# Layer 2 of a three-stage fused kernel in tiles of 1024 tokens

## The reference, cut to what matters

```python
N, C, F = 6016, 256, 2048                 # tokens, width, hidden width
qn = q / (norm(q, axis=tokens) + 1e-6);  kn = k / (norm(k, axis=tokens) + 1e-6)
a  = softmax_rows(kn.T @ qn / tau)        # 256 x 256
x  = v @ a                                # 6016 x 256
h  = x @ w_in1;   g = where(h > 0, h, exp(min(h, 0)) - 1);   x = g @ w_out1     # layer 1
h  = x @ w_in2;   g = h * sigmoid(h);                        out = g @ w_out2   # layer 2
```

## Time and profile before

| | us |
|---|---|
| time, median of 3 runs | 1018.54 (1018.07 to 1018.68) |
| the profiled execution's own time | 1018.29 |
| its span, first to last instruction | 1016.2 |
| TensorE busy in it | 1010.8 (99%) |
| VectorE busy | 790.2 (78%) |
| ScalarE busy | 572.9 (56%) |
| DMA moved | 58.86 MB, mean 58 GB/s |

### The profile page before, as it was taken

The page is one execution under the profiler, slowest core; times in us unless marked ns, Lnnn a source line. Parts: engine busy times, 40 slices in busy tenths (PEclk is TensorE's granted clock), DMA queues, the critical chain, the costliest instruction groups (busy, mean ns, idle before and its releaser), DMA issues.

```text
span 1016.2 us, 15807 instructions
## 1 busy us (share of the span) xinstructions
PE 1010.8 (99%) x5718; PEld 918.4 (90%) x5718; DVE 790.2 (78%) x1291; ACT 572.9 (56%) x926; POOL 10.2 (1%) x11
## 2 busy tenths in 40 slices
PE   9999999999999999999999999999999999999998
PEld 8888888888888888888899999999999999999998
DVE  7789878778777677776777787877878878878875
ACT  6766545555445444454445566566665665665641
POOL 0300000000000000000000000000000000000000
PEclk9999999999999999999999999999999999999999
DMA  9913202112111020110121102012022022021011
GB/s 350 367 18 73 73 24 60 63 32 73 42 21 51 13 63 41 21 57 1 42 84 73 63 1 63 16 48 62 0 62 62 0 62 62 0 62 40 14 22 37
DMA packets 109921, 58.86 MB, mean 58 GB/s; under 512 B 92208, under 2 KB 98992, under 8 KB 107056
## 3 DMA queue, kind: packets, MB, share of 16 engines
q1 hardware_dynamic: 109728, 57.95, 19.6%
q10 hardware_dynamic: 144, 0.26, 0.1%
HBM read 39.72 MB, written 18.48 MB: 57 GB/s over the span
## 4 chain that ended last, share of the span: by engine, by line
PE 98%; DMA 1%; issue 0%; DVE 0%; SPq 0%; ACT 0%; POOL 0%; DVEq 0%; POOLq 0%
PE bank L992 73%; PE bank L1124 20%; PE bank L1002 2%; PE bank L1141 2%; DMA early_w_in<-w_in 1%; PE bank L1020 0%; SPq L412 0%; ACT early_w_in_parts L341 0%; PE bank L1035 0%; PE bank L1041 0%; ACT early_scores L593 0%; DVE early_scores L787 0%; DVE small L790 0%; DVE out_tile L978 0%; SPq L489 0%
## 5 line engine op out<-in xcount | busy, mean ns | idle before, releaser
L992 PE MATMUL bank<-g_parts,w_out_parts 128*128 128x512 f32 (+1 forms) x1152 | 274.8, 375 | 0.0
L992 PE MATMUL bank<-xT_parts,a_w_in 128*128 128x512 f32 (+1 forms) x1152 | 274.3, 375 | 0.0
L992 PE MATMUL bank<-xT_parts,w_in_parts 128*128 128x512 f32 (+1 forms) x1152 | 260.6, 375 | 0.0
L652 ACT ACTIVATE g_raw<-bank 128x512 f32<-128x512 f32 (+1 forms) x192 | 112.8, 588 | 234.9 <-PE bank L992 222.1
L992 PEld LDWEIGHTS bank<-xT_parts,a_w_in 128*128 128x128 f32 x1152 | 215.7, 189 | 28.5
L992 PEld LDWEIGHTS bank<-g_parts,w_out_parts 128*128 128x128 f32 x1152 | 215.6, 189 | 28.3
L992 PEld LDWEIGHTS bank<-xT_parts,w_in_parts 128*128 128x128 f32 x1152 | 208.4, 190 | 23.5
L1124 PEld LDWEIGHTS bank<-g_pair_parts,w_out_forms 128*128 128x128 f32 x1848 | 219.9, 192 | 5.9 <-issue 1.4
L1124 PE MATMUL bank<-g_pair_parts,w_out_forms 128*128 128x256 f32 x1848 | 220.6, 275 | 1.0 <-issue 1.0
L683 ACT ACTIVATE g_pair_parts<-g_forms 128x1024 fp32r<-128x1024 f32 x88 | 93.2, 1059 | 148.0 <-DVE g_forms L902 78.9
L909 DVE TENSOR_TENSOR g_pair_parts<-g_forms,g_pair_parts 128x1024 fp32r<-128x1024 f32 x88 | 107.8, 1225 | 77.6 <-ACT g_pair_parts L683 77.6
(11 more groups left out here) (82 smaller groups left out, 401.0 us busy)
## 6 DMA issues: line engine op xcount, KB each, us to landing
y_parts<-y1T_parts SPq DMA_DIRECT2D x11, 1024.0 KB, 3.8
xT_parts<-y_parts SPq DMA_DIRECT2D x11, 1024.0 KB, 5.4
early_qk<-q SPq DMA_DIRECT2D x23, 256.0 KB, 8.0
out<-out_tile SPq DMA_DIRECT2D x45, 128.0 KB, 2.6
early_qk<-k SPq DMA_DIRECT2D x22, 256.0 KB, 8.4
v_in<-v SPq DMA_DIRECT2D x40, 128.0 KB, 3.2
early_w_in<-w_in SPq DMA_DIRECT2D x4, 512.0 KB, 10.7
early_w_out<-w_out SPq DMA_DIRECT2D x2, 1024.0 KB, 13.7
```

Source lines behind the costliest of these rows:

```text
L652: act.activation(g_sb[:, f % 2, 0:ph.n], h_ps[f % N_H][:, 0:ph.n], ACT.Exp).then_inc(u_act, 1)
L992: mm = pe.matmul(dst, lhsT, rhs, start=first and n == 0, stop=last and n == len(todo) - 1)
```

## The change

Layer 2 runs over 6 tiles: five of 1024 tokens and one of 896. Each half of a tile is one tile of layer 1. So that this fits, layer 1's last two tiles have 448 tokens each (before: 512 and 384).

- **Matmuls.** The two token halves of the seven products are now 512 tokens each (448 in the last tile), so each product has a whole bank: `m_banks` = banks 1 to 7. For h one bank is left, bank 0 (`h_bank`). An `up` waits until ScalarE has read the h before it (`u_act`). In the first tile's pairs 0 and 1, where no products run yet, h still goes round four banks.
- **Order on TensorE.** A step k of a tile has four slots. In each slot there is one `pair_up` (6 matmuls), then 5, 5, 5 or 6 of the 21 matmuls of the pair two steps back.
- **Order of ScalarE and VectorE.** In the four slots ScalarE does `sums_hi` 0 and 1 and `plain_hi` 0 and 1 of the pair before, each followed by one `silu`. The copies of the previous tile's products are shared: three on ScalarE, four on VectorE. The first tile's `silu`s of pair 0 come before the split of layer 1's last y, and VectorE's `pair_sums` of pair 0 after it.
- **The last tile** uses the seven products too. After the last matmul come the rest of the copies, the sums, four transposes and 16 stores (4 for each of the four quarters of C).
- **w_out's sums** go to DRAM in layer 1, a pair at a time (`form_spill`), and come back by pairs, 0.92 MB each, into a ring of four, in every tile (`ring_load`, 48 loads).

```diff
+PARTS_OF_SLOT = (0, 5, 10, 15, 21)
...
-        m_banks = bank[4:8]
+        m_banks = bank[1:8]
+        def h_bank(u, k, i):
+            return bank[(4 * k + i) % N_H if u is TWO[0] and k < LAG_PAIRS else 0]
 # TensorE
+            def pair_up(u, k, i):
+                f, a = 2 * k + i // 2, i % 2
...
+                ring_of_h = u is TWO[0] and k < LAG_PAIRS
+                pe.wait_ge(u_act, up_of(u, k, i) - (N_H - 1 if ring_of_h else 0))
...
+            def tile(u):
+                for k in range(PAIRS):
+                    back = shifted(u, k, LAG_PAIRS, PAIRS)
+                    for i in range(4):
+                        pair_up(u, k, i)
+                        if back:
+                            pair_down(*back, *PARTS_OF_SLOT[i:i + 2])
+                        elif k == 0 and i < LAG:
+                            down(ONE[-1], FB - LAG + i)
+            tiles_two(pe, tile)
+            for k in range(PAIRS - LAG_PAIRS, PAIRS):
+                pair_down(LAST, k, 0, N_PRODUCTS * len(PARTS))
 # ScalarE
+            def tile(u):
+                for k in range(PAIRS):
+                    back = shifted(u, k, 1, PAIRS)
+                    if u is TWO[0] and k == 0:
+                        g_hi(ONE[-1], FB - 1)
+                    for i in range(4):
+                        if back:
+                            (sums_hi if i < 2 else plain_hi)(*back, i % 2)
+                        if u.before and (k, i) in K_ACT_COPY:
+                            m_copy(u.before, M_ACT[K_ACT_COPY.index((k, i))])
+                        silu(u, k, i)
+                    if u is TWO[0] and k == 0:
+                        y1_hi_of(ONE[-1])
 # VectorE
+            def tile(u):
+                for k in range(PAIRS):
...
+                    if back:
+                        pair_sums(*back, 2)
+                        sums_lo(*back, 0)
+                        sums_lo(*back, 1)
+                    if u is TWO[0] and k == 0:
+                        y1_lo_of(ONE[-1])
+                    if u.before:
+                        for m, at_k in zip(M_DVE, K_DVE_COPY):
+                            if k == at_k:
+                                m_copy(u.before, m)
+                        for step in range(4):
+                            if k == K_SUMS[step]:
+                                c_sums(u.before, step)
...
+                    pair_sums(u, k, 0)
+                    pair_sums(u, k, 1)
+                    if back:
+                        plain_lo(*back)
...
+            for m in M_DVE[:3]:
+                m_copy(LAST, m)
+            for step in (0, 1, 3):
+                c_sums(LAST, step)
...
+            dve.tensor_tensor(mc[:, C21, 0:LAST.n], mc[:, M4, 0:LAST.n], mc[:, U3, 0:LAST.n], ALU.add).then_inc(c_out, 1)
+            for c, a in LAST_ORDER[:3]:
+                c_transpose(LAST, c, a)
+            dve.wait_ge(p_down, PAIRS * NU)
+            dve.tensor_tensor(by_w(mc[:, C12, 0:LAST.n]), m_banks[M3][:, 0:LAST.n].rearrange("p (x w) -> p w x", w=4),
+                              by_w(mc[:, U4, 0:LAST.n]), ALU.add).then_inc(c_out, 1)
+            c_transpose(LAST, *LAST_ORDER[3], done=5)
 # SyncE
+            def last_store(a, c):
+                sp.wait_ge(y2_out, 4 * (NU - 1) + LAST_ORDER.index((c, a)) + 1)
+                rows = rows_of_tile(out, NT - 2 + a, T_LAST)
+                for i in range(A):
+                    sp.dma_start(rows[i].rearrange("p (g c) i -> p g c i", c=CB)[:, :, c, :],
+                                 o_sb[i * BLK:(i + 1) * BLK, a, 0:T_LAST // BLK, c, :]).then_inc(d_out, 16)
```

More of the change, by code:

```diff
@@ L102, in place @@
             return nc.alloc_sbuf_tensor_at(name, shape, dt, offset=offset)
+        at_win2_parts = cursor[0]
+        win2 = place("w_in2_parts", [P, 2, CB, F], F32R)
+        at_xb = cursor[0]
+        xb = [[place(f"x_parts{b}{a}", [P, 2, CB, T], F32R) for a in range(2)] for b in range(2)]
+        ident = place("ident", [P, P], F32)
+        ones = place("ones", [P, P], F32)
+        small = place("small", [P, 32], F32)
         at_win1 = cursor[0]
@@ new lines, in build @@
+        gp2 = [place("g_pair_parts0", [P, 2, N_PRODUCTS, T], F32R, at_wout1),
+               place("g_pair_parts1", [P, 2, N_PRODUCTS, T], F32R, at_g)]
+        assert at_wout1 + 2 * N_PRODUCTS * T * 4 <= at_x and at_g + 2 * N_PRODUCTS * T * 4 <= at_stage
+        cursor[0] = at_x
+        ring += [place(f"w_forms{r}", [P, N_PRODUCTS, 2, P], F32R) for r in range(1, N_RING)]
+        assert cursor[0] <= at_g
+        cursor[0] = at_stage
+        mc = place("m_tile", [P, N_PRODUCTS + 2, T], F32)
@@ L280, in layer_phases, with phases_one @@
+        def phases_one(eng, one):
+            for ph in ONE[:IN_LOOP_1[0]]:
                 one(ph)
-            with eng.Fori(0, len(in_loop) // 2) as i:
-                layer, half = phases[0].layer, i + in_loop[0] // 2
-                a = Phase(layer, half, 0, before=Phase(layer, half - 1, 1))
+            with eng.Fori(0, len(IN_LOOP_1) // 2) as i:
+                half = i + IN_LOOP_1[0] // 2
+                a = Phase(half, 0, before=Phase(half - 1, 1))
                 one(a)
-                one(Phase(layer, half, 1, before=a))
@@ L729, in _ @@
+            tiles_two(act, tile)
+            for s in range(2):
+                sums_hi(LAST, PAIRS - 1, s)
+            for s in range(2):
+                plain_hi(LAST, PAIRS - 1, s)
+            for m in M_ACT:
+                m_copy(LAST, m)
         @block.vector
@@ new lines, in pair_down @@
+            def pair_down(u, k, first, end):
+                for n in range(first, end):
+                    m, part = n // len(PARTS), n % len(PARTS)
+                    (form, operand), (x, y) = PRODUCTS[m], PARTS[part]
+                    if n == 0:
+                        pe.wait_ge(d_ring[k % N_RING], 16 * (2 * u.number + k // N_RING) + 16)
+                        pe.wait_ge(t_lo, 2 * pair(u, k) + 2)
+                        if k == 0 and u is TWO[0]:
+                            pe.wait_ge(y1_lo, CB * NT)
+                    if part == 0 and k == 0 and u is not TWO[0]:
+                        if m in M_ACT:
+                            pe.wait_ge(m_act, 3 * (u.number - 1) + M_ACT.index(m) + 1)
+                        else:
+                            pe.wait_ge(m_dve, 4 * (u.number - 1) + M_DVE.index(m) + 1)
+                    if n == N_SUMS * len(PARTS):
+                        pe.wait_ge(r_lo, pair(u, k) + 1)
+                    mm = pe.matmul(m_banks[m][:, 0:u.n], ring[k % N_RING][:, form, x, :],
+                                   by_turns(gp2[k % 2][:, y, operand, 0:u.n]),
+                                   start=k == 0 and part == 0, stop=k == PAIRS - 1 and part == len(PARTS) - 1)
+                    if k == PAIRS - 1 and part == len(PARTS) - 1 and m < N_PRODUCTS - 1:
+                        mm.then_inc(m_done, 1)
+                    if n == N_PRODUCTS * len(PARTS) - 1:
+                        mm.then_inc(p_down, 1)
```

616 lines of the change are left out of this document (276 added, 340 removed).

## The result

The changed kernel takes 1027.43 us (median of 4 runs, 1026.55 to 1028.46) against 1018.31 for the kernel before: ratio 1.0091, 95% interval 1.0073 to 1.0108. The profiled execution took 1028.46 us with a span of 1026.7, 10.5 us more than the span before. In a later series the same kernel had a median of 1026.6, ratio 1.0085 (1.0071 to 1.0099). It is slower by some 9 us. 1024.0 was forecast: the direction was right, the size too small by 3.4.

The account below looks back on a forecast made before the run. TensorE, busy 99% of the span, was taken as the bound. TensorE's work -9.6, layer change +4.1 and kernel end +11.1 gave +5.6 us on 1018.3, stated as 1024.0; 8-in-10 range 1019.5 to 1032.

Parts of the forecast that it names:

- Wider products: Layer 2: 512-column products make a step 9.71 us against 9.87, 6.4 us over five tiles; TensorE's work shrinks by 9.6 in all.
- The other 3.2 us: Last tokens of layer 2: seven products instead of eight save TensorE 3.2 us.
- The 71.2 us: Layer 2 before the change: time given for the last 1408 tokens, 8 x 4.935 + 16 x 1.98 us.
- rival 4: Layer 2 products: width gains only what the skill's rule says, terms 5.1 us smaller, 1029 us; chance 0.05.
- One bank for h: Slots of layer 2: ScalarE frees bank 0 in time, 0.14 us to spare in slots of five; cost 0, at most 14 us.
- The seam: From layer 1 to layer 2: TensorE waits 4.2 us, then 1.0 more, against 1.15 before: +4.1 us, bounds 2 and 8.
- the fall of the clock: Wait between the layers: clock drops from 2.4 to 1.2 GHz, +3.5 us, 1027.5 us; chance 0.10.
- the second wait: Start of layer 2: the second up waits for a silu held by VectorE's `plain_lo` of pair 0, 1.0 us.
- The tail: After the last matmul: SyncE's 16 stores, not the sums, set the end, 13.9 us against 2.8: +11.1, bounds +8.8 and +14.6.
- the distance between two issues: Last stores on SyncE's queue: 0.50 us each with 448 runs, 15 distances after the first at 4.2 us.
- Ring loads, form spills: Layer 2's 48 loads, one per 9.71 us, and the spills stay hidden: cost 0, at most 3 us.
- Rival 3: Last stores: at 0.25 us an issue or less, transposes set the end, tail +7.2, 1018 us, not slower; chance 0.17.

Follow-up runs that it names:

- experiment 5: Changed kernel with each layer 2 product made by two matmuls of 256 columns (224 in the last tile) instead of one of 512 (448): 1041.43 us, ratio 1.0229.
- experiment 1: Changed kernel with VectorE making pair 0's sums before the split of layer 1's last y, not after: 1023.8 us, ratio 1.0059.
- experiment 4: Changed kernel with the last stores as 8 DMAs of 896 runs instead of 16 of 448, all on SyncE's queue: 1023.59 us, ratio 1.0051.

## Why the prediction was right, and where its sizes were off

- **Wider products: right in the sum, partly wrong in the reason.** 9.71 us a step was forecast and measured, and experiment 5 gives the 6.4 us of the full tiles back to the hundredth of a step. The other 3.2 us were put down to the seventh product in place of the eighth. Experiment 5 shows that they need the width too: with two matmuls of 224 columns the last tile would cost more than before. Two slips of the prediction did no harm. The 71.2 us are the time of 896 tokens, not of the last 1408. And rival 4 could hardly come true: the forecast starts from the measured time of the kernel before, where the rows have 0.1117 us for a matmul of 256 columns. The rule of the Trainium skill ("TensorE: Matmul & The Clock Gate", section "Wait — 56ns, not 53.3ns?": N / 2.4 GHz plus about 2.5 ns) holds here for 512 and 448 columns (215.8 and 189 ns). For 256 and 224 it does not: it would give 109.2 and 95.8 ns (estimates), and the traces have 111.7 and 110. The same page's section "LDWEIGHTS (loading the stationary operand)" gives a load of 128 columns 128 / 1.2 GHz = 107 ns. Together with the 2.5 ns that is an estimate of 109 ns for the floor, and the traces have 110 to 112. That the weight load makes the floor is argued, not shown.
- **One bank for h: right.** TensorE has no idle time at bank 0 in the 120 + 24 slots outside the seam. The way there and back is 0.96 us (0.94 forecast).
- **The seam: right in its place and its chain, too small.** A wait of 4.2 was forecast and 3.96 came, behind the very sum that was named. What failed was the step after it: I took TensorE to go on at full clock, and had the fall of the clock as a rival of its own with a chance of 0.10, though the forecast's own wait of 4 us was its condition. Here it should have been a term of the forecast. It cost 3.06 us in the profile, from which the second wait (1.0 forecast, 0.70 seen in experiment 1) goes off, because the slow matmuls hid it: +5.9 instead of +4.1. That the median (1027.4) lies at this rival's 1027.5 is luck: the rival adds 3.5 us to the forecast's seam, for which no row stood, and the seam was only 1.8 us dearer than forecast. The tail did the rest.
- **The tail: right in its mechanism, mis-sized.** The first store went out 4.3 us after the last matmul (4.2 forecast) and the queue, not the sums, set the end. The term of the sum that was off is the distance between two issues: 0.50 us, read from loads of v, against 0.66 measured; 15 distances are 2.4 us. Another 0.4 is the last store's way to the end (2.6 us from its issue, 2.2 forecast). The row to take was the stores' own. The line shown in experiment 4 has 0.69 from one start to the next, and with that the sum would have been 4.2 + 15 x 0.69 + 2.2 - 2.8, some +14. I had scaled it down by the number of runs, and experiment 4 shows that the runs hardly count. Tail +14.0 instead of +11.1.
- **Ring loads, form spills: right.** 4.6 us to land and no wait.
- Rival 3 (not slower, from 0.25 us an issue) did not come: one queue takes 0.66 us. Two queues together come to about 0.35 us a store, and then the DMA engines are full.

Sum of the misses: 1.8 at the seam and 2.9 in the tail, 4.7 of the 4.9 us by which the span was missed. The median was missed by 3.4, because the profiled execution was 1.0 us slower than the median of its series and the time outside the span was 0.3 us shorter than in the kernel before (1.8 instead of 2.1).

## What to carry to other kernels

A change that makes the steady state cheaper by 0.16 us a step can be undone at its two ends: count what every engine does between the last work of one stage and the first full step of the next, and what follows the last matmul. If TensorE is left waiting, look for the granted clock behind the wait and add the slow matmuls to its price; here a wait of 1.9 us was free of that, and one of 3.96 was not in five profiles of six. Price a burst of small DMAs by the number of DMAs on a queue first, then by what the DMA engines do with the run length.

## What the runs showed of the hardware that I had not expected

- Matmuls that each bring their own 128 columns of weights hardly get cheaper below 256 columns: 224 columns take 0.110 us, 256 columns 0.1117, 448 columns 0.189, 512 columns 0.2158. Nothing narrower was measured.
- With a wait of 3.96 us the clock fell to half in five profiles of six, with 1.8 to 3.1 us lost on the matmuls behind it, and stayed in the sixth. With TensorE kept busy in the same stretch it did not fall in any of five runs. After waits of 1.9, 0.81 and 0.70 us it never fell, in five profiles.
- Issuing a store of 128-byte runs costs a queue 0.66 us with 448 runs and 0.70 with 896; SyncE's and ScalarE's queues issue side by side, and with both the 16 DMA engines are full at 166 to 181 GB/s (share 1.03 and 1.13).
